# A fused clustered-attention, MoE and MLP kernel: the first pair's masks made head by head, three loads moved

## The reference, cut to what matters

```python
# q, k, v: [2, 8, 768, 64]; centroids: [8, 16, 64]
mask = argmax(q_n . c_n) == argmax(k_n . c_n)          # same cluster of 16
attn = softmax(where(mask, q k^T / 8, -1e9))
x = (attn @ v) as [1536, 512]
logits = x @ w_gate; e_idx = argmax(logits)            # 8 experts, one per token
x = gate_w * sigmoid(x @ w_output_gate) * (relu(x @ w1[e]) @ w2[e])
h = x @ w_in; out = (h * sigmoid(1.702 h)) @ w_out
```

## Time and profile before

| what | us |
|---|---|
| median of 3 runs | 767.33 |
| lowest and highest | 766.16, 768.53 |
| the profiled execution | 767.02 |
| its span, first to last instruction | 765.3 |
| PE busy in it | 737.6 (96%) |
| DVE, ACT, POOL busy | 423.1, 376.0, 168.7 |

### The profile page before, as it was taken

The page is one execution under the profiler, slowest core; times in us unless marked ns, Lnnn a source line. Parts: engine busy times, 40 slices in busy tenths (PEclk is TensorE's granted clock), DMA queues, the critical chain, the costliest instruction groups (busy, mean ns, idle before and its releaser), DMA issues.

```text
span 765.3 us, 11526 instructions
## 1 busy us (share of the span) xinstructions
PE 737.6 (96%) x4013; PEld 627.1 (82%) x4013; DVE 423.1 (55%) x789; ACT 376.0 (49%) x721; POOL 168.7 (22%) x249
## 2 busy tenths in 40 slices
PE   7899999999999998899999999999999999999996
PEld 5688999988899976678888888788888888888884
DVE  5678798889879886656565656443222212131211
ACT  3677887887877953655656565533111101010101
POOL 5324424344864950000000000004202000020002
PEclk9999999999999998999999999999999999999998
DMA  7885374553737246756445633330001000010001
GB/s 151 200 187 124 73 161 112 121 125 88 189 87 230 81 185 220 300 205 231 156 165 208 225 147 124 124 110 1 0 1 56 0 1 1 0 56 1 0 1 55
DMA packets 60157, 86.13 MB, mean 113 GB/s; under 512 B 31552, under 2 KB 33600, under 8 KB 59584
## 3 DMA queue, kind: packets, MB, share of 16 engines
q1 hardware_dynamic: 53872, 74.69, 33.6%
q0 software_dynamic: 2352, 6.31, 2.2%
q10 hardware_dynamic: 3872, 4.36, 1.9%
HBM read 55.97 MB, written 8.92 MB: 85 GB/s over the span
## 4 chain that ended last, share of the span: by engine, by line
PE 80%; DVE 5%; SPq 4%; DMA 3%; POOL 3%; issue 2%; ACT 2%; ACTq 1%; DVEq 0%; POOLq 0%
PE ps L1024 17%; PE ps L727 11%; PE ps L806 6%; PE ps L1039 5%; PE ps L1041 5%; PE ps L1040 5%; PE ps L940 4%; PE ps L941 3%; PE ps L942 3%; PE ps L953 3%; PE ps L954 3%; PE ps L955 3%; SPq L413 3%; PE ps L782 3%; PE ps L778 3%; PE ps L793 2%
## 5 line engine op out<-in xcount | busy, mean ns | idle before, releaser
L1320 ACT ACTIVATE g<-ps 128x512 f32<-128x512 f32 x48 | 28.7, 598 | 202.7 <-PE ps L1024 202.7
L1721 DVE CAST gt_h<-g 128x512 fp32r<-128x512 f32 x48 | 21.0, 438 | 178.5 <-ACT g L1320 174.6
L1450 DVE TENSOR_TENSOR pt_l<-ps,pt_h 128x384 fp32r<-128x384 f32 x192 | 98.0, 551 | 32.7 <-ACT pt_h L1147 32.1
L1406 DVE TENSOR_REDUCE nmax<-ps 128x1 f32<-128x768 f32 x96 | 91.0, 949 | 4.9 <-PE ps L782 4.9
L1147 ACT CAST pt_h<-ps 128x384 fp32r<-128x384 f32 x192 | 84.9, 487 | 16.0 <-PE ps L727 16.0
L1123 ACT ACTIVATE probs<-ps,nmax 128x768 f32<-128x768 f32 x96 | 88.3, 919 | 6.4 <-DVE nmax L1406 6.4
L727 PE MATMUL ps<-ident,probs 128*128 128x128 f32 x576 | 83.6, 276 | 2.8 <-ACT probs L1123 1.9
L1024 PE MATMUL ps<-x2t_h,wl 128*128 128x512 f32 x192 | 74.9, 390 | 1.4 <-DVE wl L1631 1.4
L727 PEld LDWEIGHTS ps<-ident,probs 128*128 128x128 f32 x576 | 65.7, 140 | 12.6 <-DVE pt_l L1450 6.6
L1024 PE MATMUL ps<-x2t_h,wh 128*128 128x512 f32 x192 | 74.8, 389 | 0.0
L1024 PE MATMUL ps<-x2t_l,wh 128*128 128x512 f32 x192 | 74.8, 389 | 0.0
(11 more groups left out here) (216 smaller groups left out, 1495.7 us busy)
## 6 DMA issues: line engine op xcount, KB each, us to landing
raw<-in_moe_w SPq DMA_DIRECT2D x32, 1024.0 KB, 6.9
ka<-hi_t SPq DMA_DIRECT2D x32, 192.0 KB, 4.2
raw<-in_moe_w_in SPq DMA_DIRECT2D x4, 1024.0 KB, 5.7
raw<-in_moe_w_out SPq DMA_DIRECT2D x4, 1024.0 KB, 6.6
xg<-xs ACTq DMA_DIRECT2D x15, 256.0 KB, 3.4
qn<-in_q SPq DMA_DIRECT2D x16, 192.0 KB, 3.7
vn<-in_v SPq DMA_DIRECT2D x8, 384.0 KB, 4.6
qa<-hi_t SPq DMA_DIRECT2D x16, 192.0 KB, 4.2
```

What stands on the lines that cost most here:

```text
L1406: nc.vector.reduce_max(nmax[:, s % 4:s % 4 + 1], halves(score_bank(s)), AX.XY, negate=True).then_inc(m_ready, 1)
L1450: nc.vector.tensor_tensor(pt_l[g % 2][at_p], ps[:, 4 + half, 0:GQ].rearrange("p (c n) -> p c n", c=GT), pt_h[g % 2][at_p].bitcast(F32), AL ...
```

## The change

In the prologue:
- SP no longer loads the gate weights before v; they come after the mask rows of head 1. After head 0's stack SP waits until it has landed, and only then loads q and k of pair 1. `mask_rows(0, 0)` is gone.
- The two casts of k's high half go from DVE to ACT; DVE makes three of the four low halves, POOL one (before: two and two).
- DVE makes head 0's part of `cval`, `cmax` and `onehot` first, at half the width, then head 1's. PE turns head 0's q and k masks each by itself into PSUM partitions 64 to 79 (`first_masks`, 12 transposes into banks 4 and 5), from where ACT writes `qb` and DVE writes `kb` directly.
- PE issues four `qa`/`ka` matmuls, then the four `qb`/`kb` ones, and only after them the full `masks(0)` that head 1 needs and the first quarter of pair 1. ACT's `mask_out(0)` comes behind the first exponential.

In `body(0)`: quarter 1 of pair 1 in slot 0, quarters 2 and 3 in slot 1 (before: one in each of slots 0 to 2); the steps that `first` had one slot late now stand where they stand in other pairs; the wait for `s_wg` is in slot 8. In a later pair (i = 5) SP's count-dependent zero fill comes behind `stack(6)`.

```diff
             load_heads(sp, q_v, qn, s_q, 0)
-            for half in range(2):
-                for n, w in enumerate((w_gate, w_output_gate)):
-                    sp.dma_start(fold[...], w.rearrange("(h d) e -> d h e", d=D)).then_inc(s_wg, 16)
             load_values(0)
-            sp.wait_ge(h_done, 2)
+            sp.wait_ge(h0_done, 2)
             query_high(0, 0)
-            sp.wait_ge(h_done, 4)
+            sp.wait_ge(h1_done, 2)
             key_high(0, 0)
             sp.wait_ge(l_done, 4)
             low_rows(0, 0)
+            sp.wait_ge(s_stack[0][0], 96)
             load_heads(sp, q_v, qn, s_q, 1)
-            sp.wait_ge(t_done, 1)
-            mask_rows(0, 0)
             load_heads(sp, k_v, kn, s_k, 1)
             query_high(0, 1)
             key_high(0, 1)
             low_rows(0, 1)
+            sp.wait_ge(t_done, 1)
             mask_rows(0, 1)
+            for half in range(2):
+                for n, w in enumerate((w_gate, w_output_gate)):
+                    sp.dma_start(fold[...], w.rearrange("(h d) e -> d h e", d=D)).then_inc(s_wg, 16)
             load_values(1)
...
                     load(i + 2)
+                stack(i + 1)
                 if i == PPB + 1:
                     sp.wait_ge(g_first, 1)
...
-                stack(i + 1)
...
+            def first_masks():
+                wait_apart(pe, oh_ready0, 1)
+                for a, bank in ((2, 5), (0, 4)):
+                    dst = ps[D:D + C, bank, 0:S // 2].bitcast(BF16)
+                    for t in range(T):
+                        last = nc.tensor.transpose(dst[:, t * P:(t + 1) * P], onehot[:, 2 * (t % GT) + t // GT, a * C:(a + 1) * C], ident_b[:, :])
+                    last.then_inc(m_ready0, 1)
...
-            idle(7)
+            idle(4)
...
-            idle(6)
-            masks(0, (c_read, 1))
-            idle(4)
-            scores(0, 0, 0, stacks=0)
-            scores(1, 1, 0)
-            transposed(1, 0, (t_done, 1))
+            idle(5)
+            first_masks()
+            idle(2)
+            pe.wait_ge(s_stack[0][0], 96)
+            (4 matmuls qa x ka: tiles 0 and 1, two halves each)
+            pe.wait_ge(s_mask[0][0], 32)
+            (4 matmuls qb x kb, s_ready after each tile)
+            masks(0, (c_read, 1))
+            transposed(1, 0, None, bank=6)
...
-                    if first and s < 3:
-                        transposed(1, s + 1, (x32_done, 4 + s + 1))
+                    if first and s == 0:
+                        pe.wait_ge(t_done, 1)
+                        transposed(1, 1, (x32_done, 5))
+                    elif first and s == 1:
+                        transposed(1, 2, (x32_done, 6))
+                        transposed(1, 3, None, bank=6)
...
-            pe.wait_ge(s_wg, 64)
...
             wide_out(0)
+            act.wait_ge(m_ready0, 2)
+            nc.scalar.copy(qb[0][0][D:D + C, :], ps[D:D + C, 4, 0:S // 2].bitcast(BF16)).then_inc(s_mask[0][0], 16)
+            exps(0, 0, 0)
+            out_32(1, 0, False, bank=6)
             mask_out(0)
-            exps(0, 0, 0)
...
+            dve.wait_ge(m_ready0, 1)
+            nc.vector.tensor_scalar(kb[0][0][D:D + C, :], ps[D:D + C, 5, 0:S // 2].bitcast(BF16), -1.0, MASKED, ALU.add, ALU.mult).then_inc(s_mask[0][0], 16)
```

More of the change, by code:

```diff
@@ L608, in low @@
             def low(n, j):
-                wait_apart(pool, h_done, 4 * n + j + 1)
+                if n == 0:
+                    wait_apart(pool, h1_done, j - 1)
+                else:
+                    wait_apart(pool, h_done, 4 * (n - 1) + j + 1)
                 cols = slice((j % 2) * GQ, (j % 2 + 1) * GQ)
@@ L620, in value_clusters @@
                 ).then_inc(c_val, 1)
-            for j in range(2):
+            for j in range(2, 3):
                 low(0, j)
@@ L672, in _ @@
             for i in range(PAIRS):
-                n, first = i + 1, i == 0
+                n = i + 1
                 for s in range(TPP):
                     g = NG * i + s // GT
-                    if n < PAIRS and s - first in range(4):
-                        high(n, s - first)
-                        low(n, s - first)
+                    if n < PAIRS and s < 4:
+                        high(n, s)
+                        low(n, s)
                     if s == 0 and i:
@@ L687, in _ @@
                     if n < PAIRS:
-                        if s == 4 + first:
+                        if s == 4:
                             value_clusters(n)
@@ L822, in _ @@
             clusters_by_token(0)
-            idle(6)
+            idle(5)
+            first_masks()
+            idle(2)
+            pe.wait_ge(s_stack[0][0], 96)
+            for tile in range(2):
+                for half in range(2):
+                    nc.tensor.matmul(ps[:, 2 * tile + half, 0:GQ], qa[0][0][:, tile * P:(tile + 1) * P], ka[0][0][:, half * GQ:(half + 1) * GQ], start=True, stop=False)
+            pe.wait_ge(s_mask[0][0], 32)
+            for tile in range(2):
+                for half in range(2):
+                    last = nc.tensor.matmul(ps[:, 2 * tile + half, 0:GQ], qb[0][0][:, tile * P:(tile + 1) * P], kb[0][0][:, half * GQ:(half + 1) * GQ], start=False, stop=True)
+                last.then_inc(s_ready, 1)
             masks(0, (c_read, 1))
-            idle(4)
-            scores(0, 0, 0, stacks=0)
-            scores(1, 1, 0)
-            transposed(1, 0, (t_done, 1))
+            transposed(1, 0, None, bank=6)
             def ranks(st):
@@ L870, in body @@
                         by_token(NG * i - 2, (xn_done, NG * i - 2) if last else (x32_done, 4 * n + 2))
-                    if s == 2 + first and not last:
+                    if s == 2 and not last:
                         clusters(n)
@@ L875, in body @@
                     if s == 8:
+                        if first:
+                            pe.wait_ge(s_wg, 64)
                         by_token(NG * i, (xn_done, NG * i) if last else (t_done, n + 1))
@@ L894, in body @@
                         transposed(n + 1, s + 2 - TPP, (xn_done, NG * i + 2) if s == TPP - 2 else (x32_done, 4 * n + 5))
-                    if s == 3 + first and not last:
+                    if s == 3 and not last:
                         clusters_by_token(n)
@@ L1159, in body @@
                         out_of_psum(g - 2, g % 2, None if g < 4 else g - 3)
-                    if first and s < 4:
-                        out_32(1, s, False)
+                    if first and s == 1:
+                        out_32(1, 1, False)
+                    elif first and s == 2:
+                        out_32(1, 2, False)
+                        out_32(1, 3, False, bank=6)
                     elif s < 3 and not first and not last:
@@ L1172, in body @@
                         exps(tile + 1, 0, 1 - par)
-                    if not last and s == 2 + first:
+                    if not last and s == 2:
                         wide_out(n)
@@ L1377, in high @@
                 cols = slice((j % 2) * GQ, (j % 2 + 1) * GQ)
[L1378 removed]
+                nc.vector.tensor_copy(hi_t[j // 2][:, cols], x32[j // 2][:, cols]).then_inc(h0_done, 1)
             def cluster_maxima(n, part):
@@ L1462, in body @@
                     probs_low(tile, 0)
-                    if s == 6 + first and not last:
+                    if s == 6 and not last:
                         pick_clusters(n)
@@ L1485, in body @@
                             gate(0)
-                    if not last and s - first in (3, 5):
-                        cluster_maxima(n, (s - first - 3) // 2)
+                    if not last and s in (3, 5):
+                        cluster_maxima(n, (s - 3) // 2)
             def choose(st, part):
```

43 lines of the change are left out of this document (33 added, 10 removed).

## The result

| | before | after |
|---|---|---|
| median of 10 runs each, us | 766.02 (764.29 to 769.33) | 770.80 (768.93 to 773.95) |
| profiled execution, us | 767.02 | 769.66 |
| its span, us | 765.3 | 767.9 |
| granted clock over that span | 0.992 | 0.993 |

The ratio is 1.0059, 95% interval 1.0041 to 1.0077: 4.8 us more. Forecast were 766.8 us, 0.5 less than the 767.33 of the first three runs of the kernel before, and a range of 765.0 to 769.9.

What follows compares the result with a forecast made beforehand. The DMA run up to the landing of pair 1's mask rows was taken to bound the kernel: 50.48 - 1.3 - 0.2 + 1.0 = 50.0, the end moving by -0.5 us, so 766.8 us by the median, range 765.0 to 769.9.

Steps and rivals of the forecast that it cites:

- q lands 0.5 earlier, head 0's stack at 17.2: Prologue: without the gate weights' small rows q lands 0.5 us earlier; with 0.2 from casts, the stack moves from 17.9 to 17.2.
- Head 0's masks by 16.2, so that the copies bind: Prologue: masks ready at 16.2, ahead of the stack at 17.2; first masked product at 17.9, 3.6 us earlier.
- Rival 3: Prologue: new PSUM reads or 12 small transposes take over 1.7 us more; still -0.5, counted within the forecast's 0.50.
- q of pair 1 is what is late next, until 21.6; second exponential 23.5; PE through with the unmasked product at 47.1: Pair 1: q, issued only at 17.2, holds PE until 21.6; its first tile's unmasked product ends at 47.1, before 49.57.
- The DMA run starts 1.3 earlier and that carries through: SP's queue: pair 0's k starts at 20.3, not 21.6, so pair 1's mask rows land 1.3 us earlier, other terms aside.
- I take 0.9 + 0.1 for the issue: 1.0: DMA run: four late gate loads add 1.0 us, 0.9 for 64 KB at 71 GB/s and 0.1 for the issue.
- as issues, behind a queue that drains: DMA run: upper price of the four gate loads, 0.85 us per issue, up to 2.7 us.
- The clock stays: Pair 1's first masked tile: no clock fall in PE's 2.9 us wait, DMA run binding, end -0.5 us; chance 0.50.
- rival 2: Pair 1's first masked tile: PE's 2.9 us wait drops the clock, costing 2.2 us: +1.7, 769.0; chance 0.28 at middling prices.
- with dear gate loads: Gate loads at their upper price (+1.7) together with the clock fall: +3.4 us, 770.7; chance 0.09.
- between 2.4 and 3 us: PE's wait length at which the clock's fall is decided; the forecast wait of 2.9 lies at its upper end.
- The end stands at the landing plus a constant: Kernel's end follows the landing of pair 1's mask rows, as PE has no wait of note until the experts.

Runs made afterwards that it cites:

- p3: The changed kernel without SP's wait for head 0's stack, gate loads still late: ratio 1.0029 to the kernel before.
- p4: Both edits: the changed kernel with the gate loads back at their early place and without SP's wait for head 0's stack: ratio 0.9999 to the kernel before.
- p5: The changed kernel with 30 products of zeros on PE ahead of pair 1's first scores: ratio 1.0055 to the kernel before.
- p8: The changed kernel with gate loads early, no SP wait for head 0's stack, seven products of zeros at the start, not four: 766.98 us, ratio 1.0008.
- p9: The changed kernel with gate loads early, no SP wait for head 0's stack, 12 products of zeros ahead of pair 1's first scores: 764.18 us, ratio 0.9975.
- p10: The changed kernel with gate loads issued by GpSimd, no SP wait for head 0's stack, 12 products of zeros ahead of pair 1's first scores: ratio 1.0003.
- p11: The changed kernel with the four gate loads behind pair 2's loads in SP's queue: 766.69 us in one execution, no ratio.
- p1: The kernel before with only the gate loads moved behind head 1's mask rows, PE waiting for them in slot 8: 769.98 us, ratio 1.0052.
- p6: The changed kernel with gate loads issued by GpSimd after its split of v, SP's wait for head 0's stack kept: ratio 1.0020.
- p2: The changed kernel with the gate loads back at their early place, between the first loads of q and v: ratio 1.0037 to the kernel before.

## Why the prediction failed, step by step

- **q lands 0.5 earlier, head 0's stack at 17.2**: q 0.86 earlier (7.16), the stack at 16.6. Right, a little better.
- **Head 0's masks by 16.2, so that the copies bind**: 16.4. Right; PE's masked products start at 17.41 (forecast 17.9). Rival 3 is out.
- **q of pair 1 is what is late next, until 21.6; second exponential 23.5; PE through with the unmasked product at 47.1**: 20.92, 22.93 and 46.45. Right.
- **The DMA run starts 1.3 earlier and that carries through**: half right. SP issued head 1's last copy 1.6 earlier (23.40). POOL too was through 1.3 earlier, at 34.80, as forecast; but SP, held up by the gate loads, came to the first copy of pair 1's stack only at 36.25, where it was issued before (36.15). With early gates q is late again, POOL is through at 35.84, and the gain at the landing was 0.8.
- **The term that failed: "I take 0.9 + 0.1 for the issue: 1.0".** The gate loads cost 2.9 us of landing alone (on the kernel before), 1.7 without SP's wait (p3 against p4), and 3.6 with it (against early gates), of which 1.8 may be the chance that p5 shows. All are above 1.0. The bound of 2.7, "as issues, behind a queue that drains", stood in the text and was the right mechanism; I chose the value from the rate of the rows, from a row in which other loads were in flight. With 2.7 the landing would have been at 51.7; measured were 53.27, and 51.45 in p5. The packet price of the Trainium skill (DMA: Bandwidth & Descriptors, "Why small descriptors are slow (HBM only)"), 0.7 us as an estimate, speaks of the transfer alone; 3.65 us of SP's time were what counted here.
- **The clock stays (0.50), or falls (rival 2, 0.28; with dear gate loads 0.09)**: it fell. Rival 2 with dear loads is what happened. That its 770.7 meets the measured 770.8 is luck: it was 3.4 us more than the 767.33 that the kernel before had in three runs, and measured were 4.8 us more than the 766.02 of ten. I gave its price as 1.7 to 2.7; measured from landing to masks 1.5 (gates early) to 2.8 (both edits). Where I was wrong is the point from which it decides, "between 2.4 and 3 us": it fell in or right behind waits of 2.31, 2.35 and 2.37 and stayed in those of 2.36, 2.58 and 3.11. The two were not independent either: dear loads lengthen the wait that drops the clock. A chance of 0.09 for both was too small.
- **"The end stands at the landing plus a constant"**: true in the profiles only where the clock is the same: 25.0 or 25.1 us without a fall in five kernels (before, p5, p8, p9, p10), 26.6 to 27.9 with one in eight.
- **Zero fill and slot 8's wait for the gates cost nothing**: right; no wait of PE for them is in the trace.

So two steps failed. The price of the gate loads, put at 1.0, was 1.7 to 3.6 at the landing; and the clock, taken to stay at 1.00 through the wait, fell, which cost 1.8 us in the changed kernel's profile. Open is why the same queue landed at 53.2 in one execution and at 51.45 in another. Not tried is the new order of the slots by itself, and a cover of p5's length fitted to its landing.

## What to carry to other kernels

Small loads were priced here by the time that the issuing engine spent on them, not by their bytes: put them where large transfers are queued ahead or where that engine waits anyway (p11, one execution), and never as the only thing between two large runs. When the start of a chain gets faster and its middle doesn't, ask how long the wait in front of the middle becomes and what it does to TensorE's clock; a dozen products of zeros there took the ratio from 0.9999 to 0.9975 (the intervals just overlap), while thirty, two microseconds more than the wait needed, brought nothing. And a profile is one execution: compare its time and clock with the other runs', and its landings with those of a kernel that has the same queue, before reading a microsecond out of it.

## What the runs showed of the hardware

- **An issue costs SP about 0.5 to 0.65 us at the least, whatever its size**: 16 KB of gate weights took 0.63 to 1.53, loads of q, 192 KB each, from 0.58 and copies of the stack from 0.46 up, most of them 0.9 to 0.97 behind one another and a few up to 1.8.
- **Waits of the same length dropped the clock in one execution and not in another.** It fell in or right behind waits of 2.31, 2.35, 2.37, 2.42, 2.79, 2.89, 2.92, 2.95, 2.96, 3.01, 3.11, 3.46, 3.83, 5.23 and 6.82 us, and stayed through 2.36, 2.58, 2.92, 2.95, 2.96 (the covered changed kernel, at 296), 2.98, 3.06 and 3.11. Four of these lengths are on both sides, and 2.35 and 2.36 are the same wait at 17 us in p1 and in the kernel before. In p6 and p11 it also fell at 20.7 and 20.5 us, within single waits of 1.2 and 1.4 us (granted clock 0.67 and 0.63 from 20 to 22); what that cost was not measured by itself. The granted clock was then 0.50, 1.2 GHz, for 3 to 6 us after work had resumed, and a fall at pair 1's masked product cost 1.5 to 2.8 us, more where more of the work behind it ran at 0.50 (1.5 in p2, with a mean of 0.66 from 49 to 54, and 2.8 in p4, with 0.50). That the clock comes back only after work agrees with the Trainium skill (TensorE: Matmul & The Clock Gate, "What's actually happening"), by which activity releases it; with products of zeros in the place of the wait it stayed at 1.00.
- **A hole in the transfers at 28 us was felt 20 us later**: 724 KB less moved there in the changed kernel, DMA shares of 0.94 and 1.06 behind it left little to make up for it, and the mask rows landed 2.75 us later than before, 1.0 in p5.
